# Moving the low part of the values, the state's decay and four transposes to other places of a fused recurrence and expert kernel

## The reference

```python
for t in range(S):                                   # attention: B, H, S, D = 4, 8, 768, 48
    cur = einsum('bhd,bhe->bhde', u * k[t], v[t])
    y[t] = einsum('bhd,bhde->bhe', r[t], state + cur)
    state = w[t][:, None] * state + einsum('bhd,bhe->bhde', k[t], v[t])
x = y as [3072 tokens, 384]
h = x @ w_in                                         # 384 -> 2048
x = (h * clip(h + 3, 0, 6) / 6) @ w_out              # 2048 -> 384
logits = x @ phi                                     # 32 slots
d = softmax of logits over the tokens                # dispatch
slot_out = for each of 8 experts: relu(d.T @ x @ w1) @ w2
out = (softmax of logits over the slots) @ slot_out
```

## Time and profile before

| | |
|---|---|
| median of 3 runs | 410.31 us (410.25 to 410.34) |
| profiled execution | 410.12 us |
| its span, first to last instruction | 408.4 us |
| granted TensorE clock, mean | 0.992 |
| busy: PE / DVE / ACT / POOL | 391.8 / 330.9 / 199.8 / 217.5 us |
| DMA | 69.36 MB, mean 170 GB/s |

### The profile page before, as it was taken

One profiled execution on the slowest core, in us unless ns is written; L12 is line 12 of the kernel. 1 busy time (PEld: TensorE's weight loads), 2 busy tenths in 40 slices (PEclk: granted clock), 3 DMA queues, 4 the chain that ended last, 5 costly groups with the idle time before them and its releaser, 6 DMA issues.

```text
span 408.4 us, 10082 instructions
## 1 busy us (share of the span) xinstructions
PE 391.8 (96%) x3977; PEld 210.4 (52%) x3977; DVE 330.9 (81%) x536; ACT 199.8 (49%) x413; POOL 217.5 (53%) x206
## 2 busy tenths in 40 slices
PE   8999999999999999999999999999999999999981
PEld 3885555555555555555554555455543444543430
DVE  7998799998989898998989998989877886661251
ACT  3576356545555657365555646653443234321141
POOL 2444988978568677747785677875740012010000
PEclk9999999999999999999999999999999999999996
DMA  8999413439242144214431330342007199779929
GB/s 235 332 405 324 143 31 98 125 123 362 80 127 82 48 125 129 93 38 125 126 103 28 127 117 24 114 128 59 2 2 309 21 414 400 240 285 414 388 113 354
DMA packets 16542, 69.36 MB, mean 170 GB/s; under 512 B 2160, under 2 KB 3184, under 8 KB 14832
## 3 DMA queue, kind: packets, MB, share of 16 engines
q1 hardware_dynamic: 16496, 68.73, 48.6%
HBM read 64.00 MB, written 4.72 MB: 168 GB/s over the span
## 4 chain that ended last, share of the span: by engine, by line
PE 29%; POOL 29%; issue 27%; DMA 5%; DVE 4%; ACT 1%; SPq 1%; POOLq 0%; DVEq 0%
DMA att<-rkT_dram 5%; PE hid L617 4%; POOL att L1697 4%; PE hid L619 4%; PE hid L618 4%; POOL att L1641 4%; POOL att L1643 4%; POOL att L1670 3%; POOL att L1701 3%; POOL spare L1705 3%; PE hid L887 3%; POOL att L1662 3%; POOL w_split L1655 2%; PE inc_ps L728 1%; POOL att L1685 1%
## 5 line engine op out<-in xcount | busy, mean ns | idle before, releaser
L617 PE MATMUL hid<-x_split,w_split 128*128 128x512 f16 x285 | 108.3, 380 | 0.7 <-DVE gated L1076 0.7
L1474 ACT ACTIVATE relu<-hid,three 128x512 f32<-128x512 f32 x95 | 65.0, 684 | 88.1 <-PE hid L619 88.1
L619 PE MATMUL hid<-x_split,w_split 128*128 128x512 f16 x285 | 108.0, 379 | 0.0
L618 PE MATMUL hid<-x_split,w_split 128*128 128x512 f16 x285 | 108.0, 379 | 0.0
L1076 DVE SCALAR_TENSOR_TENSOR gated<-relu,hid 128x512 f32<-128x512 f32 x95 | 64.2, 676 | 21.5 <-ACT relu L1474 21.1
L1097 DVE STREAM_TRANSPOSE ring<-gated 128x512 f32<-128x512 f32 x96 | 68.3, 711 | 3.3
L1676 POOL TENSOR_TENSOR att<-att 128x1024 f16<-128x1024 f32 x20 | 42.1, 2104 | 34.9 <-ACT att L1381 34.9
L617 PEld LDWEIGHTS hid<-x_split,w_split 128*128 128x128 f16 x285 | 27.7, 97 | 37.1 <-issue 7.1
L619 PEld LDWEIGHTS hid<-x_split,w_split 128*128 128x128 f16 x285 | 27.8, 98 | 33.7
L1685 POOL TENSOR_TENSOR att<-att 112x512 f32<-112x512 f32 x21 | 25.5, 1213 | 36.5 <-DVE att L976 26.9
L618 PEld LDWEIGHTS hid<-x_split,w_split 128*128 128x128 f16 x285 | 27.9, 98 | 24.7
(11 more groups left out here) (300 smaller groups left out, 862.3 us busy)
## 6 DMA issues: line engine op xcount, KB each, us to landing
att<-nat_dram SPq DMA_DIRECT2D x20, 576.0 KB, 4.3
att<-rkT_dram SPq DMA_DIRECT2D x22, 448.0 KB, 5.7
att<-wT_dram SPq DMA_DIRECT2D x22, 226.2 KB, 4.7
att<-w_dram SPq DMA_DIRECT2D x3, 1536.0 KB, 9.7
out_dram<-w_split SPq DMA_DIRECT2D x11, 384.0 KB, 3.9
att<-w_dram SPq DMA_DIRECT2D x5, 768.0 KB, 10.5
stage<-w_in_dram SPq DMA_DIRECT2D x2, 1536.0 KB, 14.6
ring<-w_outT_dram SPq DMA_DIRECT2D x1, 3072.0 KB, 16.6
```

Source lines behind the costliest of these rows:

```text
L617: pe.matmul(hid[s % 2][:], high, x_high, start=(q == 0), stop=False)
L618: pe.matmul(hid[s % 2][:], high, x_low, start=False, stop=False)
L619: last = pe.matmul(hid[s % 2][:], low, x_high, start=False, stop=(q == KT - 1))
L1474: nc.scalar.activation(relu_tile(s), hid[s % 2][:], ACT.Relu, bias=three[:], scale=GATE / H_SCALE)\
```

## The change

Four edits.

- DVE: low_v(n) for n = 5, 6, 7 moves from phase 2 (s = 3, 7, 11) to phase 0 (s = 1, 5, 9), behind add_state(n - 1) and so ahead of gate(s). At s = 1 gate(1) and its transpose stand ahead of both.
- The decay of the state for units 5, 6, 7 (at s = 0, 4, 8) goes from POOL, one instruction, to ACT, four (decay_old_state, ahead of relu_step). diag_values for units 5, 6, 7 (s = 4, 8, 12) go from POOL, one instruction, to ACT, eight (loop_diag_values, behind relu_step).
- DVE: turn_logits(2) moves from s = 57 to s = 53, phase 0, behind add_state.
- DVE: turn_gated(80) moves from the end of s = 80 to s = 82, where turn_gated(81) was, ahead of turn_weight(4), and turn_gated(81) moves to s = 83, ahead of sum_weight(4).

```diff
--- before.py
+++ after.py
@@ -1235,7 +1235,9 @@
                         finish_y(n - 1)
                     if n - 1 < LAST_INC:
                         add_state(n - 1)
-                    if 1 <= g < C - 2 and i == 9:
+                    if B < n < SPLIT:
+                        low_v(n)
+                    if (g, i) in ((1, 9), (2, 9), (3, 5)):
                         turn_logits(g - 1)
                 if phase == 1:
                     if 1 <= g < C and i == 2:
@@ -1252,11 +1254,13 @@
                         low_x(n - 1)
                     if 1 <= g < C and i == 2:
                         if g == C - 1:
-                            turn_gated(s - 1)
+                            turn_gated(s - 2)
                         turn_weight(g - 1)
                     if g == C and i == 2:
                         last_maximum()
                 if phase == 2:
+                    if s == STEPS - FT + 3:
+                        turn_gated(s - 2)
                     if g == C and i == 3:
                         turn_weight(C - 1)
                     if g >= 1 and i == 3:
@@ -1265,8 +1269,6 @@
                         low_x(n - 1)
                     if is_unit(n):
                         sum_diag(n)
-                    if n < SPLIT:
-                        low_v(n)
                 if s == 0:
                     sum_diag(B)
                     low_w(1)
@@ -1304,7 +1306,7 @@
                     gate(s)
                 if s == STEPS - FT - 1:
                     turn_logits(C - 3)
-                if 1 < s < STEPS - 2 and s != STEPS - FT + 1:
+                if 1 < s < STEPS - 2 and s not in (STEPS - FT, STEPS - FT + 1):
                     turn_gated(s)
                 if s == STEPS - 1:
                     last_gate(0)
@@ -1410,6 +1412,25 @@
                     last = nc.scalar.activation(s, s, ACT.Copy, scale=chunk_decay[n % B][0:PD, p:p + 1])
                 last.then_inc(decayed, 1)
 
+            def decay_old_state(n):
+                act.wait_ge(suffix_done, n + 1)
+                act.wait_ge(state_copied, n - B + 1)
+                for p in range(PB):
+                    s = state[n % B][0:PD, p, :]
+                    first = 1 + p * (P + 1)
+                    last = nc.scalar.activation(s, s, ACT.Copy, scale=suffix[0:PD, first:first + 1])
+                last.then_inc(decayed, 1)
+
+            def loop_diag_values(n):
+                act.wait_ge(diag_done, n + 1)
+                act.wait_ge(y_done, n)
+                if n >= SPLIT:
+                    act.wait_ge(v_scaled, n - SPLIT + 1)
+                for h in range(H):
+                    cols = slice(h * D, (h + 1) * D)
+                    last = nc.scalar.activation(diag_v[:, cols], nat_of(n, 2)[:, cols], ACT.Copy, scale=diag[:, h:h + 1])
+                last.then_inc(diag_v_done, 1)
+
             def high_receptance(n):
                 act.wait_ge(r_dec_done, n + 1)
                 act.wait_ge(y_ready, n)
@@ -1576,6 +1597,8 @@
                         save_decay(n + 1)
                     if SPLIT - B <= n - 2 < LAST_INC:
                         high_state(n - 2)
+                if phase == 3 and n + 1 < SPLIT:
+                    decay_old_state(n + 1)
                 if phase == 3 and SPLIT <= n - 1 < LAST_INC:
                     decay_new_state(n - 1)
                 if s < STEPS - 1:
@@ -1585,6 +1608,8 @@
                         last_relu(half)
                 if s == 0:
                     copy_keys(B)
+                if phase == 3 and B < n < SPLIT:
+                    loop_diag_values(n)
                 c = scaled_behind(s)
                 if c is not None:
                     high_w(c)
@@ -1763,10 +1788,8 @@
                         decay_receptance(n + 1)
                     elif B < n and n + 1 < UNITS:
                         decay_keys(n + 1)
-                    if is_unit(n) and n > B:
+                    if is_unit(n) and n >= SPLIT:
                         diag_values(n)
-                    if n + 1 < SPLIT:
-                        decay_state(n + 1)
                     if SPLIT - B <= n - 2 < LAST_INC:
                         low_state(n - 2)
                 c = split_behind(s)
```

## The result

The changed kernel takes 408.41 us (median of 6 runs, 408.12 to 409.11 but for one) against 410.28 for the kernel before: ratio 0.9956, 95% interval 0.9942 to 0.997, which is 1.9 us less; forecast were 408.7 and 1.6 less. The whole interval lies beyond the 0.2% named in the forecast.

A forecast was written before the change was run, and what follows sets the result against it. The prediction took TensorE, busy 391.8 of 408.4 us, as the bound, leaving 16.6 us idle. Terms +0.24 - 0.71 - 1.22 + 0.8 - 0.35 - 0.48 + 0.09 = -1.63 us gave 408.7 us; range 407.6 to 409.8.

The forecast's parts named there:

- Sum: Whole kernel: the seven terms add to -1.63 us, giving 408.7 us against the median of the runs.
- attend(4): At attend(4): relu(0) slips behind the decay on ACT, low_v(4) loses the port to low_scores(4); cost +0.24 us.
- s = 81 to 86: Late transposes: the 0.48 us stall at fold_logits goes but is given back by mlp(86); +0.09 in all.
- Part 1: Units 6 and 7: low_v two steps earlier ends the stalls before attend(6) and attend(7), -0.71 and -1.22 us.
- Both stalls go: -0.71 and -1.22 us: At attend(6) and attend(7): v_lo is ready at least six microseconds before, so neither stalls.
- the new wait: At increment(6): copy_keys(6) comes late because low_v(6) waits for low_w(4) on POOL; +0.8 us.
- the prediction's 0.07 us: In unit 6: low_w(4), at 59.44, is 0.07 us ahead of low_v(6), at 59.51, and takes the port.
- rival 1: In unit 6: low_v(6) takes the port first, no stall at increment(6); -2.43 us, 407.9 us; chance 0.28.
- Part 2: Units 5 to 7: decays and diagonal values go from POOL to ACT, which mostly has idle time for them.
- costs nothing: On ACT: the decays at s = 4 and 8 lie in idle time (1.96 us); a later relu costs nothing.
- Unit 7: No stall at increment(7), 0.3 us to spare; the stall before mlp(12) goes, low_v no more ahead of gate(10): -0.35.
- Parts 3 and 4: turn_logits(2) to s = 53 wins 0.48 us at mlp(64); turn_gated(80) and (81) later, +0.09.

The follow-up runs named there:

- the first experiment: The changed kernel, unaltered, timed again and profiled at full clock: 408.66 us, ratio 0.9946 against the kernel before.
- low_v back: The changed kernel with low_v at its old place in DVE's queue: 408.32 us, ratio 0.9954 against the kernel before.
- the relief of POOL alone: The kernel before with only decays and diagonal values moved from POOL to ACT, low_v at its old place: 408.81 us, ratio 0.9954.
- the move alone: The kernel before with only low_v moved, decays and diagonal values staying on POOL: 409.51 us, ratio 0.9977.
- high_v sooner: The changed kernel with high_v(6) and high_v(7) on ACT ahead of the diagonal copies of the step before: 407.72 us, ratio 0.995.
- the first decay back: The changed kernel with the decay of unit 5 left on POOL: 407.37 us, ratio 0.9933 against the kernel before.
- turn_gated back: The changed kernel with turn_gated(80) and (81) where they were: 408.61 us, ratio 0.9963 against the kernel before.
- the late transposes: The kernel before with only turn_logits(2), turn_gated(80) and (81) moved: 410.05 us, ratio 0.9998.
- the decay version: The kernel before with only the decays of units 6 and 7 moved to ACT: 409.14 us, ratio 0.9982.
- the version with turn_logits(4) behind gate(84): Changed kernel, high_v(6), high_v(7) sooner, unit 5's decay on POOL, turn_logits(4) and its maximum behind gate(84): 408.05 us, ratio 0.995.

## Why the prediction was right, and where it was not

**Sum.** Term by term, forecast and measured in starts of steps: attend(4) +0.24, +0.2; attend(6) -0.71, -0.72; attend(7) -1.22, -1.23; increment(6) +0.8, +0.85; mlp(12) -0.35, -0.34; mlp(64) -0.48, -0.51; s = 81 to 86 +0.09, +0.03. Sum -1.63, and -1.68 from step 0 on. The median moved by 1.87 and in the first experiment by 1.75.

**Part 1, low_v: sizes right, cause read one link deep.** The step that fails is "Both stalls go: -0.71 and -1.22 us" as the effect of the move. The stalls go in the changed kernel, but with the move undone 0.30 us of them come back (low_v back), and with the relief of POOL alone 0.41 and nearly all of the 1.22 go. low_v's 1.44 us are a wait for POOL's low_w, as the prediction reads them. It did not ask why low_w was there so late, though the scans in DVE's queue, at 2.05 and 2.73 us for 1.22, and POOL's low_scores, at 2.59 and 2.93 for 2.00, were longer than others of their kind in the same way. The forecast for the changed kernel came out because I replayed its queues with both edits in them; that the relief without the move would do nearly the same, it did not say. The forecasts for the edits taken singly, made from the booked cause, missed: 1.0 us at the move alone, and the sign at the relief alone.

**Part 1, the new wait: right.** increment(6) waits for copy_keys behind mask_scores behind low_v(6) behind low_w(4). Three ways to take that wait away gave the same 0.8 us (low_v back, high_v sooner, one instruction more on POOL), so this is shown. The Trainium skill's rule, "SBUF — State Buffer", section "Who interferes with whom" (the first to issue has the shared pair for the whole instruction), agrees with the trace in that the loser waits for the winner's end: low_v(6) took 2.02 us with low_w(4) in front, and 0.74 with low_w(4), stretched from 1.65 to 1.98, behind it (the first decay back). Who the winner is can be read from the starts of rows only roughly (last section), and the prediction's 0.07 us were far less than that allows. That the forecast came and not rival 1 was luck; the prediction gave the two 0.45 and 0.28.

**Part 2: "costs nothing" was half of it.** The decays of units 6 and 7 on ACT do lie in idle time, and the copies make relu(5) late without loss. The step that failed is what the part left out of the sum: a gain. That unloading POOL is worth more than the move of low_v (1.74 against 0.69 us in starts of steps, each alone) is missing: the relief counts only in the place of low_w(4), 1.58 us sooner. The 0.2 us at attend(4) was right and is the price of the decay of unit 5 on ACT.

**Unit 7, mlp(12): right, for the wrong reason.** I gave "low_v is no more behind it in the queue" first and POOL second. It is POOL: the relief alone has the 0.34, the move alone 0.14.

**Parts 3 and 4: right.** mlp(64) won 0.51 where 0.48 was forecast, and turn_gated brought no net gain, with the same two rows giving it back. Rival 1 (low_v(6) first) did not come, but one instruction more or less on POOL or ACT brings it about, at 0.8 us.

## What to carry to other kernels

A wait booked on an instruction can be the end of a chain: before moving the instruction, look in its own queue and in that of the engine it shares a port with for rows that last longer than others of their kind, and follow them back to the first. When two engines exclude each other, what matters is what lies in front of the critical one in the other's queue, and an instruction taken off the uncritical engine can be worth more than one moved on the critical. Here, a transpose pushed along a queue without idle time was only given back at the next gate.

## What the runs showed of the hardware

Three things. First, the order in which the rows of DVE and POOL start does not by itself say which of the two got the port. DVE's and POOL's timeline with only low_v moved:

```profile
59.10 0.55 DVE L1045 TENSOR_TENSOR att<-att,inc_ps 112x384 f32<-112x384 f32 x1
59.56 0.55 DVE L1060 SCALAR_TENSOR_TENSOR att<-att 128x384 f16<-128x384 f32 x1
...
59.28 1.71 POOL L1641 TENSOR_TENSOR att<-att 128x384 f32<-128x384 f32 x1
```

Here POOL's row starts 0.28 us ahead of low_v(6)'s and low_v still takes its 0.55, POOL's 1.71 instead of 1.01; with high_v sooner the lead was 0.46, and it was the same. In both low_v follows another DVE instruction directly. That is not enough to win. The scan of unit 6 in the changed kernel follows mask_scores(5) as directly, and lost at a lead of 0.22 us, waiting to 1.09 behind the end of POOL's row:

```profile
47.98 2.50 DVE L985 TENSOR_TENSOR_SCAN att<-att 112x517 f32<-112x517 f32 x1
...
47.76 1.64 POOL L1680 TENSOR_TENSOR w_split<-stage,w_split 128x768 f16<-128x768 f32 x1
```

Scans lost at 0.47 us too (62.49 against 62.02, only low_v moved) and at 0.70 (62.35 against 61.65, kernel before). And where low_v(6) came out of a wait for ACT, as in the changed kernel, it lost at 0.04 us (0.03 in the profile with turn_gated back, where PE's 0.79 us are the same) and won when its row was 0.29 us in front. Whether a queued DVE instruction asks before its row starts, or POOL after its row starts, these runs don't tell; POOL's rows are rough. So a gap under half a microsecond in a timeline did not tell the winner here, though 0.8 us of PE's time hung on it.

Second, the start has a lottery of its own. From 20.4 to 30.6 us the DMA engines move 405 GB/s by the page of the kernel before, more than in all but two other slices of its forty, and in some executions the transfer of w for unit 5 lands late. PE, and DVE's scan of the suffix, in the profile of the late transposes:

```profile
44.79 0.43 PE L576 MATMUL y_ps<-att 112*128 112x96 f32 x2 [2.71 <-POOL att L1678]
...
36.23 1.24 DVE L985 TENSOR_TENSOR_SCAN att<-att 112x517 f32<-112x517 f32 x1 [1.23 <-DMA att<-wT_dram]
```

The scan waits 1.23 us for the transfer, decay_keys(5), diag_products(4) and low_scores(4) on POOL follow, and attend(4) has 2.71 us of idle time instead of 0.59. This execution took 413.53 us; the one of the decay version, with 0.79 us at the same scan, took 413.94. The other long executions were not profiled, so whether they are of this kind is not shown. What makes the transfer late in some executions I did not find out.

Third, the idle time is not the whole loss. Step 1 loses 3.64 us in the first of these executions, of which 2.12 are idle time; from the start of attend(4) to mlp(2) PE then takes 5.43 us instead of 3.90. Its granted clock, 1.00 while it stood idle, is 0.50 from 45.5 to 48.3, the lower of its two levels (1.2 GHz instead of 2.4), and a quarter of attend(4) takes 0.78 us from start to start instead of 0.43. In the decay version PE is idle for 2.17 us before attend(4), the clock is 0.50 from 44.5 to 50.5, and the same stretch takes 6.86 us: there the clock costs 2.96 us and the idle time only 1.58 more than before. In the version with turn_logits(4) behind gate(84), where PE is idle for 1.16 us at the same place, the clock stays at 1.00.
